# Loading and splitting the first two heads of a threshold-attention kernel piece by piece, over two DMA queues and three engines

## What is computed

```
attention, for each of 4 x 8 heads, 576 tokens, head size 64 (all f32):
    scores = (q @ k.T) / 8
    keep scores >= max(row) - tau, set the others to -1e9
    attn   = exp(scores - max(row)), divided by its row sum
    x      = attn @ v                                  # heads side by side: 4 x 576 x 512
token mixing and perceptron:
    u = x + (x.T @ U @ V).T ;  x = u + relu(u @ w_ch1) @ w_ch2
gated output:
    out = (sigmoid(causal 5-tap convolution of x) * (x @ w_val)) @ w_out
```

## Time and profile before

| what | us |
|---|---|
| median of three runs (lowest, highest) | 852.21 (850.66, 853.07) |
| the profiled execution | 852.96 |
| its span in the profile | 851.2 |

### The profile page before, as it was taken

The page is one execution under the profiler, slowest core; times in us unless marked ns, Lnnn a source line. Parts: engine busy times, 40 slices in busy tenths (PEclk is TensorE's granted clock), DMA queues, the critical chain, the costliest instruction groups (busy, mean ns, idle before and its releaser), DMA issues. The chain is left out here.

```text
span 851.2 us, 18586 instructions
## 1 busy us (share of the span) xinstructions
PE 826.3 (97%) x6864; PEld 771.5 (91%) x6864; DVE 451.0 (53%) x996; ACT 401.3 (47%) x1019; POOL 396.2 (47%) x290
## 2 busy tenths in 40 slices
PE   5999999999999979999999999999999999999998
PEld 4888888888888859999999999999999999989987
DVE  6899999999999845332241322323223223375231
ACT  5899999999999943321121211212111112244231
POOL 4998777677771100046082360733707338092000
PEclk9999999999999989999999999999999999999999
DMA  7544334433332002200000000000000102032221
GB/s 179 123 115 111 82 83 110 123 92 82 82 99 61 12 17 87 85 1 29 1 1 30 1 29 1 2 28 1 29 1 1 53 14 82 10 123 94 90 78 62
DMA packets 27731, 48.98 MB, mean 58 GB/s; under 512 B 5344, under 2 KB 14112, under 8 KB 27680
## 3 DMA queue, kind: packets, MB, share of 16 engines
q1 hardware_dynamic: 24944, 43.54, 18.4%
q10 hardware_dynamic: 2736, 4.72, 1.5%
HBM read 38.81 MB, written 8.85 MB: 56 GB/s over the span
## 5 line engine op out<-in xcount | busy, mean ns | idle before, releaser
L888 DVE SCALAR_TENSOR_TENSOR h_lo<-psum,h_hi 128x288 fp32r<-128x288 f32 x128 | 58.6, 458 | 244.3 <-ACT h_hi L813 244.3
L813 ACT ACTIVATE h_hi<-psum 128x288 fp32r<-128x288 f32 x128 | 52.7, 412 | 255.4 <-PE psum L749 255.4
L747 PE MATMUL psum<-u_split,w_hi 128*128 128x288 f32 x512 | 152.1, 297 | 3.1 <-PEq L167 3.1
L749 PE MATMUL psum<-u_split,w_lo 128*128 128x288 f32 x512 | 152.2, 297 | 0.0
L748 PE MATMUL psum<-u_split,w_hi 128*128 128x288 f32 x512 | 151.8, 297 | 0.0
L529 DVE SCALAR_TENSOR_TENSOR probs<-psum,thresh,exp_scores 128x576 f32<-128x576 f32 (+1 forms) x160 | 128.9, 806 | 8.2 <-ACT exp_scores L398 2.2
L520 DVE TENSOR_REDUCE neg_max<-psum 128x1 f32<-128x576 f32 (+1 forms) x160 | 120.5, 753 | 17.5 <-PE psum L286 14.3
L958 POOL TENSOR_TENSOR conv<-x_t,cw 128x576 f32<-128x576 f32 x14 | 16.1, 1152 | 232.6 <-DVE x_t L896 232.0
L398 ACT ACTIVATE exp_scores<-psum,neg_max 128x576 f32<-128x576 f32 (+1 forms) x160 | 117.6, 735 | 0.0
L285 PE MATMUL psum<-qk_split 128*128 128x288 f32 (+1 forms) x320 | 106.0, 346 | 10.4 <-DVE qk_split L508 9.4
L747 PEld LDWEIGHTS psum<-u_split,w_hi 128*128 128x128 f32 x512 | 97.0, 189 | 3.9 <-issue 3.3
(11 more groups left out here) (125 smaller groups left out, 1855.2 us busy)
## 6 DMA issues: line engine op xcount, KB each, us to landing
qk_raw<-in_qk SPq DMA_DIRECT2D x60, 288.0 KB, 4.2
out<-o_sb ACTq DMA_DIRECT2D x18, 256.0 KB, 2.0
w_stage<-in_w SPq DMA_DIRECT2D x16, 256.0 KB, 2.7
v_main<-in_v SPq DMA_DIRECT2D x16, 256.0 KB, 2.7
conv<-in_w SPq DMA_DIRECT2D x16, 256.0 KB, 2.7
conv_dram<-conv SPq DMA_DIRECT2D x7, 576.0 KB, 2.8
gates<-conv_dram SPq DMA_DIRECT2D x7, 576.0 KB, 3.8
probs<-in_qk SPq DMA_DIRECT2D x4, 288.0 KB, 4.8
```

Of the source, the lines that this page charges most:

```text
L747: nc.tensor.matmul(out, w1_hi[:, cols], u_hi[:, half, d], start=(d == 0), stop=False)
L749: mm = nc.tensor.matmul(out, w1_lo[:, cols], u_hi[:, half, d], start=False, stop=(d == DB - 1))
```

## The change

The first two heads are still loaded into probs, but at columns of its slots 1 and 2, and in pieces: query rows 0 to 127 of both heads (FIRST), all keys of head 0 and of head 1 (KEYS), and query rows 128 to 575 of both heads (REST). SP issues tau, FIRST, keys of head 1, REST, and then what it issued before; ScalarE's queue issues the keys of head 0, where it issued tau before. VectorE and ScalarE split FIRST and the keys; POOL splits REST, one head after the other (scale, round, subtract), ahead of its work on head 2. TensorE waits for POOL's rest_split before query block 1 of each of the two heads. The three small VectorE instructions of the threshold now come before the split. The bytes loaded are the same.

```diff
-    first_in = [sem(f"first_in{i}") for i in range(2)]
+    first_k_in = [sem(f"first_k_in{i}") for i in range(2)]
+    first_q_in = sem("first_q_in"); rest_q_in = sem("rest_q_in")
+    first_q_hi = sem("first_q_hi"); rest_step = sem("rest_step"); rest_split = sem("rest_split")
...
+    def first_heads(part, cols):
+
+        start = (S if part else 0) + cols.start
+        return probs[:, 1:3, start:start + cols.stop - cols.start]
+
+    FIRST, REST, KEYS = slice(0, Q_ROWS[0]), slice(Q_ROWS[0], S), slice(0, S)
...
-            for a in range(2):
+            def load_first(part, cols, a, done):
                 for h in range(2):
-                    sp.dma_start(probs[D * h:D * h + D, a].rearrange("p (a b) -> p a b", a=2),
-                                 qk[a]).then_inc(first_in[a], 16)
+                    sp.dma_start(first_heads(part, cols)[D * h:D * h + D, a],
+                                 qk[a, :, part, cols].rearrange("a d s -> d a s")).then_inc(done, 16)
+
+            sp.dma_start(tau_sb[:], tau).then_inc(tau_in, 16)
+            load_first(0, FIRST, slice(0, 2), first_q_in)
+            load_first(1, KEYS, slice(1, 2), first_k_in[1])
+            load_first(0, REST, slice(0, 2), rest_q_in)
...
             pool.wait_ge(tau_ready, 1)
+            pool.wait_ge(rest_q_in, 32)
+            for hd in range(2):
+                q_in, hi = first_heads(0, REST)[:, hd], split[:, hd, 0, REST]
+                cols = [P, S - Q_ROWS[0]]
+                nc.gpsimd.tensor_tensor(q_in, q_in, q_scale[:].broadcast_to(cols), ALU.mult).then_inc(rest_step, 1)
+                pool.wait_ge(rest_step, 2 * hd + 1)
+                nc.gpsimd.tensor_tensor(hi, q_in, one[:].broadcast_to(cols), ALU.mult).then_inc(rest_step, 1)
+                pool.wait_ge(rest_step, 2 * hd + 2)
+                nc.gpsimd.tensor_tensor(hi[D:P], q_in[D:P], hi[D:P].bitcast(F32), ALU.subtract).then_inc(rest_split, 1)
+                pool.wait_ge(rest_split, hd + 1)
...
                 if b == 0 and t is None and pair == 0:
                     pe.wait_ge(first_split, a + 1)
+                elif b == 1 and t is None and pair == 0:
+                    pe.wait_ge(rest_split, a + 1)
...
-            act.dma_start(tau_sb[:], tau).then_inc(tau_in, 16)
+            for h in range(2):
+                act.dma_start(first_heads(1, KEYS)[D * h:D * h + D, 0], qk[0, :, 1]).then_inc(first_k_in[0], 16)
...
+            act.wait_ge(q_scaled, 1)
+            nc.scalar.copy(split[:, 0:2, 0, FIRST], first_heads(0, FIRST)).then_inc(first_q_hi, 1)
             for hd in range(2):
-                act.wait_ge(first_in[hd], 32)
-                nc.scalar.copy(split[:, hd, 1], probs[:, hd, S:2 * S]).then_inc(first_hi, 1)
-                act.wait_ge(q_scaled, hd + 1)
-                nc.scalar.copy(split[:, hd, 0], probs[:, hd, 0:S]).then_inc(first_hi, 1)
+                act.wait_ge(first_k_in[hd], 32)
+                nc.scalar.copy(split[:, hd, 1], first_heads(1, KEYS)[:, hd]).then_inc(first_hi, 1)
...
-            for hd in range(2):
-                hi, q_in, k_in = split[:, hd], probs[:, hd, 0:S], probs[:, hd, S:2 * S]
-                dve.wait_ge(first_in[hd], 32)
-                nc.vector.tensor_scalar(q_in, q_in, q_scale[:], None, ALU.mult).then_inc(q_scaled, 1)
-                dve.wait_ge(first_hi, 2 * hd + 1)
-                nc.vector.tensor_tensor(k_lo[:, hd], k_in, hi[:, 1].bitcast(F32), ALU.subtract)
-                dve.wait_ge(first_hi, 2 * hd + 2)
-                nc.vector.tensor_tensor(hi[D:P, 0], q_in[D:P], hi[D:P, 0].bitcast(F32),
-                                        ALU.subtract).then_inc(first_split, 1)
...
+            q_first, q_hi = first_heads(0, FIRST), split[:, 0:2, 0, FIRST]
+            dve.wait_ge(first_q_in, 32)
+            nc.vector.tensor_scalar(q_first, q_first, q_scale[:], None, ALU.mult).then_inc(q_scaled, 1)
+            dve.wait_ge(first_q_hi, 1)
+            nc.vector.tensor_tensor(q_hi[D:P], q_first[D:P], q_hi[D:P].bitcast(F32), ALU.subtract)
+            for hd in range(2):
+                dve.wait_ge(first_hi, hd + 1)
+                nc.vector.tensor_tensor(k_lo[:, hd], first_heads(1, KEYS)[:, hd], split[:, hd, 1].bitcast(F32),
+                                        ALU.subtract).then_inc(first_split, 1)
```

## The result

The changed kernel takes 855.52 us (median of 7 runs, 855.05 to 857.77) against 852.21: ratio 1.0049, 95% interval 1.0036 to 1.0061. A second comparison gave 854.46 us (6 runs) against 852.05, ratio 1.0044 (1.0029 to 1.0058). The ratios aren't those of the medians; these are 3.31 us (0.39%) and 2.41 us (0.28%) apart. One execution of the kernel before in the second comparison took 1130.27 us at a granted clock of 0.66, a slow state, and isn't used. The forecast was 855.2 us, slower by 0.36%, in a range of 852.8 to 856.8.

A forecast was written before the change was run, and what follows sets the result against it. Attention was taken as bound by engines handing units round in fixed order with little air. Start shift of 0.5 to 1.5 hidden, w1 piece 1 +3.05: 852.2 + 3.05 = 855.2 us, 0.36% slower, range 852.8 to 856.8.

The forecast's parts named there:

- The path: Near 45 us: late POOL delays SP's issue of w1 piece 1, ScalarE waits, TensorE behind it; +3.05 us.
- start shift: Start of attention: TensorE 0.5 to 1.5 us later, taken as 1.0, hidden inside ScalarE's wait for piece 1.
- The slack: w1 piece 1 lands at 44.1, ScalarE reads it at 44.61: 0.5 us to spare.
- rival 1: At 45 us: piece 1 comes in time or nearly; +2.0 (854.2) or only +1.0 (853.2); chance 0.37.
- The delay: POOL starts head 2 at 14.8 us instead of 11.10, 3.7 late, with no pause until 50 us.
- The start: First blocks: first maximum near 8.6 instead of 11.19, but unit 3 at 14.85 instead of 13.87, losing 1.0 us.
- rival 2: Start: early rest_split 2 keeps the lead of units 0 to 2; 850.5 or 849.6 us; faster, chance 0.04.
- The clock: Matmul switch to 2.4 GHz near 22 us may come one step later, 0.45 us; a longer wait covers it.
- Which queue carries what: Loads at the start: REST lands at 8.4 us by bytes or 8.2 by issue; 8.4 taken.

The follow-up runs named there:

- REST shared: Changed kernel, but VectorE and ScalarE split head 0's REST and POOL only head 1's; ratio 1.0019 of the kernel before.
- before, POOL 6: Kernel before plus 6 dummy multiplications on POOL ahead of head 2; 854.57 us, ratio 1.0028.
- changed, again: Changed kernel, unchanged, profiled a second time, in the second comparison with the kernel before; 854.46 us, span 852.1.
- changed, third: Third profile of the changed kernel, unchanged; 856.73 us, span 854.9.
- before, POOL 8: Kernel before plus 8 dummy multiplications on POOL ahead of head 2; 856.42 us, ratio 1.0056.
- one queue: Changed kernel, but the keys of head 0 are issued on SP's queue too; its one execution took 858.34 us.
- The kernel before, again: Kernel before, unchanged, run and profiled once more as a control; median 851.89 us, ratio 0.9999.
- Experiment 5: Changed kernel with REST's split divided among POOL, VectorE and ScalarE: 1.0019 of the kernel before alone, 0.9974 with w1 rounded one step later.
- experiment 4: The run one queue: changed kernel with head 0's keys on SP's queue; REST landed at 9.82 against 8.72, 858.34 us.
- the later rounding: ScalarE rounds each w1 piece one step later: 1.0002 in the kernel before; 1.0015 of before in the changed kernel.
- with w1 later: REST shared with ScalarE also rounding each w1 piece one step later; 849.6 us, ratio 0.9974 of the kernel before.

## Why the prediction was right, and where it was off

**The path: right.** POOL's work for the first heads is not paid where it is done but 30 us later, at the one place where SP's fixed order turns POOL's lateness into a late transfer. The profile of the kernel before did not show that wait; it showed only the order and how near the two times were. Seven profiles, of five kernels, in which ScalarE waits there agree within 0.4 us on one number, the time from POOL's start of head 2 to the rounding of the piece. The last column is the time of the rounding less the offset of steps 8 to 76 in the first table:

| kernel | head 2 on POOL | piece rounded | between | ScalarE waits | rounded less offset |
|---|---|---|---|---|---|
| REST shared | 12.40 | 44.38 | 31.98 | 1.41 | 44.71 |
| before, POOL 6 | 14.41 | 46.44 | 32.03 | 1.82 | 43.37 |
| changed, again | 14.99 | 47.15 | 32.16 | 1.73 | 44.72 |
| changed, third | 15.03 | 47.01 | 31.98 | 2.34 | 43.26 |
| changed | 15.18 | 47.36 | 32.18 | 1.97 | 44.71 |
| before, POOL 8 | 15.96 | 48.17 | 32.21 | 2.85 | 44.71 |
| one queue | 16.28 | 48.63 | 32.35 | 2.70 | 43.26 |

The last column is 44.7 in the four profiles whose clock stays at 1.00 behind the wait, whatever their start shift (+0.7 in two, -1.8 in another). So once ScalarE waits, the landing alone sets how late all steps behind it are, and the start shift is hidden, as foreseen. In the three whose clock falls it is 43.3 to 43.4: they lose 1.3 to 1.5 us more.

**The slack: mis-sized, 0.5 for 1.4.** By that number the piece was there at 11.10 + 32.1 = 43.2 in the kernel before. I took 44.1 from one landing of 4.5 us. The changed kernel has, for the same transfer:

```profile
43.69 0.58 SPq L201 DMA_DIRECT2D w_stage<-in_w  x1
```

```profile
w_stage<-in_w SPq DMA_DIRECT2D x1, 256.0 KB, 3.5
```

The kernel before, again, has 3.5 as well, and an issue of 0.58 where the first profile had 1.26:

```profile
39.66 0.58 SPq L192 DMA_DIRECT2D w_stage<-in_w  x1
```

The other twelve profiles have 3.3 to 3.7 for it. So the landing on which the slack rested was an outlier; rival 1 had named the odd issue as the weak spot. **The delay: 4.1 for 3.7.** REST landed at 8.7, not 8.4; POOL's pieces took 0.93, 0.93 and 1.13 us (foreseen 0.93, 0.93, 1.14 at the upper end, and I took less). The two errors go opposite ways: 4.08 - 1.4 = 2.7 us, measured +2.64 at step 7, where 3.05 was foreseen. The sum came out right in part because they cancel, and that the median (855.52) lies within 0.3 us of the forecast is luck besides: the medians of the two comparisons are 3.31 and 2.41 us apart, and the clock is in both.

**The start: right in kind.** The maxima of units 0 to 2 early, unit 3 late by 1.29 (foreseen 0.98), the start shift 0.57 to 0.71 in three of four profiles (foreseen 0.5 to 1.5); in the fourth it is -0.06. The prediction put the switch of the matmuls in the kernel before near 22 us; the transposes of step 3 take 0.60 us already at 20.46, so it was nearer 20.4. The lead in the first maximum, 2.41 us, was foreseen at 2.6.

**Faster, rival 2: wrong place, right idea.** I put it out of reach since it needed REST 2 us earlier. Experiment 5 reaches it by dividing the split instead.

**The clock: underrated.** I let the wait "cover" it. It covers a late switch at the start, but a fall can come behind the wait itself: behind waits of TensorE of 1.83, 2.36 and 2.73 us the granted clock fell to 0.50, until 52 to 54 us, and the steps lost 1.3 to 1.5 us. The first comparison gives 0.49%, and the steps of its profile, in which the clock stayed behind the wait, 2.7 us, 0.32%. Whether falls behind the wait make the difference isn't shown: the profiled execution took 855.74 us, more than the median, without one, but with the fall at 762 us; and the executions that were only timed don't show where their clock fell. The Trainium skill (TensorE: Matmul & The Clock Gate, Part 1) has idle time bring the slow level back; the rows at 0.50 behind the wait agree with it.

**Which queue carries what: by issue, not by bytes.** The prediction had both sums, 8.4 by bytes and 8.2 by issue; experiment 4 shows that the second is the one that holds, with the last issue at 4.6 us instead of 4.3 and the landing at 8.7. The Trainium skill (DMA: Bandwidth & Descriptors, Rules for kernel authors) says that a second issuing engine adds no bandwidth and saves issue time only. Experiment 4 agrees on what it saves, and the saving is worth 1.1 us here.

Open: why some executions lose the clock behind the wait and others don't. The rows show only that four of the seven profiles with a wait have the clock at 1.00 behind it and three (before with 6, one queue, the third of the changed kernel) do not; the length of the wait doesn't sort them, since TensorE waited 1.43, 1.74, 1.98 and 2.87 us in the four. And whether a second staging tile for w1, or piece 1 issued ahead of raw for head 7, would do as well as the later rounding wasn't tried.

## What to carry to other kernels

Before giving work to an idle-looking engine, find when it is next idle and what hangs on it until then; POOL was busy without a break from 11 to 52 us, and what it did there was late by the same 4 us (its first w1 low part 40.77 instead of 36.70). Follow also the queue that waits for that engine, with all that is issued behind the waiting instruction: the price here was paid by a transfer of other data. And read a slack from more than one transfer; where a consumer can be moved one step later for nothing (1.0002 here), that is cheaper than being right about 0.5 or 1.4 us.

## What was not expected of the hardware

POOL and VectorE slow each other in some pairs of instructions. In the shared version POOL's rounding of 448 columns takes 1.42 us (1.25 with w1 later) where it overlaps VectorE's subtraction with two inputs in SBUF, against 0.93 in the changed kernel, beside a row maximum that reads PSUM:

```profile
9.70 1.42 POOL L247 TENSOR_TENSOR qk_split<-probs,one 128x448 fp32r<-128x448 f32 x1
9.70 0.62 DVE L552 TENSOR_TENSOR qk_split<-probs,qk_split 64x448 fp32r<-64x448 f32 x1
```

and beside the dummies VectorE's own subtractions for head 1 grow from 0.76 us to 1.01 and 1.18, which moved unit 1 from 10.70 to 11.37:

```profile
9.12 1.01 DVE L512 TENSOR_TENSOR k_lo<-probs,qk_split 128x576 fp32r<-128x576 f32 x1 [0.18 <-ACT qk_split L455]
10.14 1.18 DVE L514 TENSOR_TENSOR qk_split<-probs,qk_split 64x576 fp32r<-64x576 f32 x1
```

A dummy, in turn, takes 0.72 us in the median and up to 1.12 (shortest, median and longest in ns):

```profile
L230 POOL TENSOR_TENSOR scratch<-one,q_scale x8: 718/718/1118, 8.6 to 15.2; 128x320 f32<-128x320 f32 x8
```

The late unit 1 alone doesn't explain the +0.59 and +0.33 of steps 0 to 6 in the table: with 6 dummies unit 1 is as late (11.42) and the steps are at -0.11, with the matmuls 0.13 us apart from 18.1 us on, against 20.9 and 20.3 with 8.
